# One VectorE product instead of two in the first attention pass, and a re-ordered second pass

## What is computed

```python
def _attn_ref(r, k, v, w, a, b):           # 4 batches, 8 heads, 768 positions, width 40
    for t in range(S):
        y[:, :, t] = einsum('bhd,bhde->bhe', rt, state)
        Sa = einsum('bhde,bhe->bhd', state, at)
        state = state * wt[:, :, None, :] - einsum('bhd,bhe->bhde', Sa, bt)
        state = state + einsum('bhd,bhe->bhde', vt, kt)

def reference(**kwargs):
    x = _attn_ref(...)                     # as 3072 tokens of 320 features
    x = _moe_ref(x, w_gate, w1, w2)        # best of 8 experts: 320 -> 1024 -> 320
    return _moe2_ref(x, w_in, w_out, alpha)  # dense: 320 -> 2048 -> 320
```

## Time and profile before

| | us |
|---|---|
| runs, median (lowest to highest) | 1080.39 (1077.92 to 1081.74) |
| the profiled execution, its own time | 1083.37 |
| its span in the trace | 1081.6 |
| first pass | 0 to 135 |
| crossing | 135 to 145.2 |
| second pass | 145.2 to 385 |
| router, experts and dense layers | 385 to 1081.6 |

### The profile page before, as it was taken

How to read it: one execution, slowest core, us unless ns; L and a number is a source line. 1 busy time by engine, 2 the same in 40 slices (tenths; PEclk the granted TensorE clock), 3 DMA queues, 4 the chain that set the end, 5 groups by cost and what they waited for, 6 DMA issues and landing times. The chain is left out here.

```text
span 1081.6 us, 47466 instructions
## 1 busy us (share of the span) xinstructions
PE 974.9 (90%) x21177; PEld 853.5 (79%) x21178; DVE 605.9 (56%) x981; ACT 316.1 (29%) x737; POOL 285.7 (26%) x351
## 2 busy tenths in 40 slices
PE   3425879999999998999999999979999999999997
PEld 3425769889888866888878888848999999999997
DVE  8896957898988761111211111146656565655655
ACT  5434645655555500011010010031121222222211
POOL 1008989798910003116611100051101000000000
PEclk9999977999999989999999999999999999999999
DMA  6877656998888537996884544320010101010100
GB/s 230 227 176 213 212 162 196 248 262 254 255 248 260 159 116 252 318 307 216 249 274 160 163 160 162 117 79 25 25 25 25 25 1 25 1 25 2 25 1 25
DMA packets 119984, 159.61 MB, mean 148 GB/s; under 512 B 60164, under 2 KB 91028, under 8 KB 119540
## 3 DMA queue, kind: packets, MB, share of 16 engines
q1 hardware_dynamic: 105636, 125.12, 38.5%
q0 software_dynamic: 5824, 25.28, 7.8%
q10 hardware_dynamic: 8464, 8.43, 2.4%
HBM read 133.15 MB, written 19.23 MB: 141 GB/s over the span
## 5 line engine op out<-in xcount | busy, mean ns | idle before, releaser
L1102 DVE TENSOR_SCALAR ht<-h_bank 128x512 f32<-128x512 f32 x62 | 42.8, 691 | 233.4 <-PE h_bank L1079 233.3
L1365 ACT CAST g_hi<-g 128x512 fp32r<-128x512 f32 x96 | 59.6, 620 | 278.6 <-DVE g L1319 278.6
L1090 PE MATMUL y_bank<-w_all,ht 128*128 x496 | 140.4, 437 | 0.3 <-DVE ht L1102 0.3
L1090 PEld LDWEIGHTS y_bank<-w_all,ht 128*128 128x128 f32 x496 | 92.7, 192 | 35.6 <-issue 1.9
L1234 PE MATMUL y_bank<-w_out_hi,g_hi 128*128 128x320 f32 x380 | 118.0, 311 | 1.4 <-DVE g_lo L1299 1.4
L1079 PE MATMUL h_bank<-xt,w 128*128 128x128 f32 x992 | 119.0, 278 | 0.0
L1234 PE MATMUL y_bank<-w_out_hi,g_lo 128*128 128x320 f32 x380 | 117.5, 309 | 0.0
L1234 PE MATMUL y_bank<-w_out_lo,g_hi 128*128 128x320 f32 x380 | 117.3, 309 | 0.0
L1079 PEld LDWEIGHTS h_bank<-xt,w 128*128 128x128 f32 x992 | 113.1, 192 | 3.8
L1221 PE MATMUL h_bank<-xt_hi,w_in_hi 128*128 128x512 f32 x288 | 113.8, 395 | 0.5 <-DVE xt_hi L1282 0.5
L1221 PE MATMUL h_bank<-xt_hi,w_in_lo 128*128 128x512 f32 x288 | 112.6, 391 | 0.0
(11 more groups left out here) (207 smaller groups left out, 1763.4 us busy)
## 6 DMA issues: line engine op xcount, KB each, us to landing
w<-w_in SPq DMA_DIRECT2D x31, 1024.0 KB, 5.9
t_in<-wab_in SPq DMA_DIRECT2D x24, 776.0 KB, 6.2
t_in<-wak_in SPq DMA_DIRECT2D x24, 776.0 KB, 6.7
w_all<-w_in POOLq DMA_DIRECT2D x8, 1280.0 KB, 8.9
rr<-rr_in SPq DMA_DIRECT2D x24, 384.0 KB, 3.3
w_rest<-w_in SPq DMA_DIRECT2D x62, 128.0 KB, 3.1
vt<-vt_in SPq DMA_DIRECT2D x24, 256.0 KB, 3.9
vtm<-vtm_in SPq DMA_DIRECT2D x24, 240.0 KB, 3.4
```

The lines of the kernel that those rows point to most:

```text
L1090: last = pe.matmul(y_bank[s][:, 0:FEAT], ht[s][:, f, :], w2[:, ds(e * W2 + f * FEAT, FEAT)], start=f == 0, stop=f == NF - 1)
L1102: dve.tensor_scalar(ht[s][:, FH * n:FH * n + FH, :].rearrange("q f t -> q (f t)"), h_bank[s][n][:, :], 0.0, None, ALU.max).then_inc(s_relu, 1)
L1365: act.copy(g_hi[j % RING][:, :], g[j % 2][:, :]).then_inc(s_ghi, 1)
```

## The change

It has four parts.

1. **First pass.** `suf` and `wq` become parts of one buffer `scans`, `alpha` and `second` of one buffer `products`. In the first pass `wq` has two slots, and one DVE instruction (128x1024) makes both products. SP and PE wait for its one semaphore.
2. **Crossing.** `alpha` is made before `second`, and both before the small copy of the totals. ACT issues the two `ax` DMAs, ahead of its copies. The five `warm` products become four, two of them ahead of the wait for `bt`.
3. **Second pass.** PE: `m1` moves from behind `z` to ahead of `eye`, `kv` behind `z`, and `mk` from behind `g2` to behind `kv`. DVE: `gates_of` before `y_out`, `alpha` once `w` is done (not `ktm`), `second` behind the scan, `m1` before the sum `w_tm`; its copy of the totals goes to ACT. ACT: `off` in halves, one before `sa` and one at the step's end; the other copies in the order shown below.
4. **SP in the second pass.** `wqx` has three slots and crosses one step earlier; `rr` is loaded in two parts; the four loads of `inv_in` go from the middle of a step's list to its end, behind the 776 KB of `t_in`.

```diff
-        suf = ring("suf", 2, [PARTS, HS, WIDE])
-        wq = ring("wq", 3, [PARTS, HS, WIDE])
-        wqx = ring("wqx", 2, [PARTS, HP, WIDE])
-        alpha, second = (m_.sb(n, [PARTS, HS, C]) for n in ("alpha", "second"))
+        scans = m_.sb("scans", [PARTS, 5, HS, WIDE])
+        wq, suf = [scans[:, s] for s in range(3)], [scans[:, 3 + s] for s in two]
+        wqx = ring("wqx", 3, [PARTS, HP, WIDE])
+        products = m_.sb("products", [PARTS, 2, HS, C])
+        alpha, second = (products[:, n] for n in two)
...
-                if k >= 1:
-                    sp.wait_ge(did["m2"], k)
-                sp.dma_start(rr[:, :, :], inp["rr"][k]).then_inc(s_vt_rr, 16)
+                for part, last in ((slice(HS, HS + HP), "st"), (slice(0, HS), "m2")):
+                    if k >= 1:
+                        sp.wait_ge(did[last], k)
+                    sp.dma_start(rr[:, part, :], inp["rr"][k][:, part, :]).then_inc(s_vt_rr, 16)
...
-            sp.wait_ge(s_alpha0, 1)
-            for h in two:
-                sp.dma_start(ax[rows(h)], alpha[rows(1 - h), HP:HS, :]).then_inc(s_ax_vtm, 16)
...
-            def scaled(j, sem):
+            def scaled(j):
+                dve.wait_ge(s_wq, j + 1)
+                first = scans[:, j % 2, :, 0:C]
+                by = bass.AP(first.tensor, first.offset, [first.ap[0], (3 * W_COLS + 2, 2), (WIDE, HS), (1, C)])
+                src = t_in[j % TR][:, W_COLS:].rearrange("q (n p t) -> q n p t", n=2, t=C)
+                dve.tensor_tensor(products[:, :, :, :], src, by, ALU.mult).then_inc(s_second, 1)
...
-            scaled(STEPS, s_alpha0)
+            dve.wait_ge(s_wq, STEPS + 1)
+            scaled_alpha(STEPS, s_alpha0)
+            scaled_second(STEPS)
+            with_total(STEPS)
...
             act.wait_ge(s_zero, 1)
-            off_diagonal(0)
+            cross_alpha(0)
+            for h in two:
+                off_diagonal(0, h)
             prepare(0)
...
+            warm(BC, 2)
             pe.wait_ge(out_of["bt"], STEPS + 1)
-            warm(2)
+            pe.wait_ge(s_second, STEPS + 1)
             pe.wait_ge(s_alpha0, 1)
             heads(with_alpha(second), BC, C, done="g2")
-            warm(3)
+            warm(BB, 2)
```

160 lines of the change are left out of this document (89 added, 71 removed).

## The result

The changed kernel takes **1087.38 us** (median; 1081.31 to 1097.14), the kernel before in the same comparison 1080.06 (1073.14 to 1088.63). The ratio is 1.007, with a 95% interval from 1.0045 to 1.0095: slower by 0.7%, where 0.75% faster was forecast (1072.3 us, with a range of 1064 to 1081). The profiled execution took 1090.4 us, its span is 1088.7.

The account below looks back on a forecast made before the run. DVE was taken to pace the first pass; in the second PE was nearly always at work, with two stands a step. Gains of 0.8 + 2.5 + 0.3 + 4.5 = 8.1 us gave a median of 1072.3 us, range 1064 to 1081.

Parts of the forecast that it names:

- SP's list: SP's issues in the second pass: reordered loads, including `inv_in` with 1.2 us of slack, land in time; cost 0.
- a new fall of the clock: Rival: the earlier start brings a new fall of PE's granted clock, landing at 1080 us; chance 0.04.
- The second pass: Steps 2 to 23: 17 steps gain 0.41 us each, 5 early ones lose 0.5 each; 4.5 us gained.
- First pass, 0.8 us: DVE's merged product saves 0.07 us a step where no load wait follows; 0.8 us, between 0 and 1.7.
- Crossing, 2.5 us: Between the passes: `ax` issued earlier by ACT lands 3.5 us later, so PE starts the second pass 2.5 us sooner.
- Steps 0 and 1, 0.3 us: Start of the second pass at lowered clock: PE is so slow that answers come in time; 0.3 us gained.
- Late steps, 9.03 us: Undisturbed second-pass steps: PE's two stands shrink and a new 0.16 us wait comes; 9.44 becomes 9.03 us.
- Early steps, 9.9 to 10.0 us: Second pass, steps 3 to 7: `gates_of` ahead of `y_out` waits for `picked`, making each step 0.5 us longer.
- The first rival: Second pass: `inv_in` lands late behind `t_in`, delaying `picked` and `y_out`; same (0.14) or slower, about 1088 (0.10).

Follow-up runs that it names:

- after: The changed kernel itself, all four parts of the change against the kernel before; ratio 1.007, median 1087.38 us.
- d_low32: d_best with `off` and `sa_tm` cut to their 32 live rows again in `z`; 1077.5 us in one execution.
- d_warm: d_best with six `warm` products instead of two ahead of the second pass; ratio 0.9982 against the kernel before.
- e_best: Changed kernel with `y_out` ahead of `gates_of`, `inv_in` between `rr` and `t_in`, the scan's wait first in the first pass; ratio 0.9961, median 1078.05 us.
- c_inv_rr: Changed kernel with `y_out` ahead of `gates_of` and the loads of `inv_in` between `rr` and `t_in`; ratio 0.9936 against the kernel before.
- d_best: c_inv_rr with the scan's wait first in the first pass and `rr` loaded whole behind `m2`; ratio 0.9967 against the kernel before.
- e_after: The changed kernel once more, unaltered (the repeat), on another chip; ratio 1.0045 against the kernel before.
- a_both: Changed kernel with `inv_in` loads back ahead of `rr` and `y_out` back ahead of `gates_of`; ratio 1.0007 against the kernel before.
- d_less: d_best without the last 256 KB of `t_in` in the second pass; 1069.9 us in one execution.
- b_cross: Kernel before with the changed crossing alone (`alpha` first, `ax` issued by ACT), `warm` products left as they were; 1089.5 us in one execution.

## Why the prediction was wrong, step by step

The step that failed is the one that put the loads at nothing: SP's list at 0 and a new fall of the clock at a chance of 0.04, with every load in time while the steps get shorter. The second pass was to gain 4.5 us and lost 6.8. In the profile of after late loads, the stands for `yt` and the falls of the clock behind both took 22.1 us beyond 22 free steps.

- **First pass, 0.8 us: too small.** The duration (1.22), the overlap (1.14) and the price per element were right for the free steps, and yet these gain nothing: unspoken was that the merged instruction starts as soon as `second` did. It has one wait more to pass behind the scan, and in this order that costs 0.08 us. In the other order a free step gains its 0.07. What the sum lacked are the last five steps: it took the 0.69 us of an early product for all 24, though the earlier trace rows has one of 0.95 at 105.91, and there the merge gains 2.2 to 2.4 us. The fixed cost of the Trainium skill (VectorE: DVE Perf Modes, "The TRN2 errata — SBUF-src ops pay a fixed extra latency per instruction"), an estimate of 0.16 us a step, isn't what a merge saves in a free step: two instructions overlap as the earlier trace rows show.
- **Crossing, 2.5 us: right by chance.** PE started 3.9 us sooner in the profile, but `alpha` ended 4.6 us sooner than before (134.28 against 138.91). Of that some 1.2 are its new place ahead of `second` and of the small copy, 2.2 the merged product in the last five steps, and the rest scatter: three profiles with the old first pass have 138.91, 139.82 and 135.66 there, two of the changed one 134.28 and 136.38. `ax` took 7.0 us instead of the 3.5 of the earlier trace rows. I took a landing time from a moment when `t_in` had been under way for 6 us, for one when it had just been issued. Alone, the crossing gave nothing. That 3.6 us were forecast up to `yt` of step 2 and 3.5 came is luck: too little for the first pass, too much for the crossing.
- **Steps 0 and 1, 0.3 us: about right.** 31.0 us from the start to `yt` of step 2, 30.5 before. The clock fell earlier, came back and fell again.
- **Late steps, 9.03 us: 8.81.** `m1` in front of `eye`, `kv` and `mk` behind `z` did what the walk through the order said, and no stand is left between `u` and `sa`. I had overlooked in the diff that `z` now multiplies 64 rows; that gives 0.15 between two groups and 0.10 of a step (d_low32).
- **Early steps, 9.9 to 10.0 us: 9.67** where no load is late. The mechanism was right, and its price 0.2 us a step instead of 0.5. With late loads these steps were 10.3 to 11.9.
- **SP's list, 0: the step that failed, with the clock below.** I counted 1.9 us for the four issues of `inv_in` wherever they stand, and 2.8 to land. Behind `t_in`, `blk` and `tt_mid` they took 3.5 to 5.8, in the other steps 1.9 to 2.9. The first rival named this mechanism with a chance of 0.24, but argued with the landing time alone; that an issue can hold SP, and with it `vt`, `vtm` and `rr`, I did not see. Nor that steps of 8.8 us instead of 9.44 ask the same 2.2 to 2.4 MB of the engines in less time, whose share was 0.83 to 0.94 already. (By the page's DMA issues a step moves 776 KB of `t_in`, 256 of `vt`, 256 of `rr`, 240 of `vtm`, 160 of rows, 132 of `wqx` and 128 each of `ax`, `inv_in` and `tt_mid`, 2204 in all, and 128 more while `blk` is loaded.)
- **The clock, 0.04 for a new fall: four of them** in the second pass, three in the repeat. I looked for falls in steps 0 and 1 only, and took the long waits of the earlier trace rows as the size that counts. Here stands of 0.7 to 2.0 us had a fall within 2 us of them, which lasted 3.4 or 6.8 us and cost at most half of that. The Trainium skill (TensorE: Matmul & The Clock Gate, "Why this matters for your kernels") warns of idle gaps between products; the trace agrees in kind and not in size, for the gaps that it warns of are longer than these.

With the third of `t_in` left out the forecast of the second pass comes out to 0.6 us: 204.0 against 209.1 - 4.5 = 204.6. That is luck too. By the measured lengths, 17 steps of 8.81 and 5 of 9.67 make 198.1, so the terms on PE were too small by 6.5 us together, and the late loads and the one fall that were left in that execution made up for it.

What is shown: without 256 KB of a step's bytes the second pass of the changed kernel is 7.9 to 11.9 us shorter (204.0 against 211.9 and 215.9), while that of the kernel before is not shorter at all (209.8 against 209.1 and 209.5). The order of `gates_of` costs 0.2 us in each early step and some of the stands, and the order of two waits 0.07 us in a free step of the first pass. By the table above the stands and the falls of the clock have about equal parts in the loss of after, 11.5 and at most 11.9 us. Late loads come without falls (d_warm, e_best: 6 us of stands, none); in the second pass of no profile were there falls without stands. Not shown is what decides whether a stand is followed by a fall, nor how many of the falls would go if only the bytes went.

## What to carry to other kernels

When PE's steps get shorter, lay the bytes of a step beside the new length first: at a DMA share near 0.9, 7% off the step (9.44 to 8.81) turned loads with slack into late ones here. In a queue that one engine issues in order, what stands behind the large load pays for it, also in the issue itself; put small loads with a deadline ahead of it, but behind the store that they depend on. And where a merged instruction meets two waits, wait first for what comes last in the stream of its own engine. Price such an instruction in each part of the stage where its rows differ, not by the first row alone.

## What the runs showed of the hardware

- One issue of a DMA took 0.43 us or up to 4.37 us (`vt` in c_inv_rr), by what had been issued before it and not by its own size; four in a row took 1.7 or 5.8.
- DVE starts a 128x1024 product 0.03 us or 0.11 us behind the scan that it depends on, by the order in which its two waits stand; with a single wait, in the first step, it was 0.03 or 0.04.
- With POOL busy for 94% of the time (108 to 134 us) two 128x512 products of DVE took 1.96 us up to the next scan and one of 128x1024 took 1.32; with POOL idle 1.21 and 1.14.
- The granted clock fell from 1.00 to 0.50 (2.4 to 1.2 GHz) behind stands of PE of 0.7 and 0.85 us (after, 311.59 and 313.59), of 0.91 (c_inv_rr, 331.06), of 1.04 (d_best), 1.16 (e_after) and 1.63 (after), but not behind one of 1.25 (e_best, 178.14), of 1.92 (a_both, 278.58) nor of 2.36 (d_less, 139.25). The length of a stand alone doesn't decide it. In the five profiles with the old second pass, where PE stood nowhere longer than 0.48 us, the clock was at 1.00 from 176 to 376, but for the tail of the long fall in b_cross.
- A group that multiplies 32 rows of 64 takes 0.61 us to the next one, and 0.46 with all 64 (d_low32, d_best).
